# Delta-rule attention and two MLP layers on one core: second half of the sequence written in backward order by the attention itself

## The reference, cut to what matters

```
attention: B, H, S, D = 4, 8, 768, 48
  for t in range(S):                     # state: D x D for each batch and head
      y[t] = q[t] @ state                # the state before key t
      state += beta[t] * outer(k_n[t], v[t] - k_n[t] @ state)
x = y as (B, S, H*D)                     # H*D = 384
layer 1: u = x + (x^T U V)^T;  x = u + relu(u @ w1) @ w2
layer 2: u = x + real(fft2(x)); un = layernorm(u); out = u + relu(un @ w1') @ w2'
```

## Time and profile before

| | us |
|---|---|
| median of 3 runs | 1141.85 |
| lowest and highest | 1141.83, 1143.81 |
| the profiled execution | 1141.97 |
| its span (first to last instruction) | 1140.2 |
| PE busy in the span | 1078.5 (95%) |
| DVE busy | 553.1 (49%) |
| ACT busy | 400.1 (35%) |
| POOL busy | 167.3 (15%) |

### The profile page before, as it was taken

One profiled execution on the slowest core, in us unless ns is written; L12 is line 12 of the kernel. 1 busy time (PEld: TensorE's weight loads), 2 busy tenths in 40 slices (PEclk: granted clock), 3 DMA queues, 4 the chain that ended last, 5 costly groups with the idle time before them and its releaser, 6 DMA issues.

```text
span 1140.2 us, 23939 instructions
## 1 busy us (share of the span) xinstructions
PE 1078.5 (95%) x10258; PEld 1025.4 (90%) x10258; DVE 553.1 (49%) x1094; ACT 400.1 (35%) x759; POOL 167.3 (15%) x213
## 2 busy tenths in 40 slices
PE   2699999999999858999999999999999999999998
PEld 1589889888988848999999999999999999999998
DVE  5677777777777315342232234265334434424222
ACT  1566767666666313231111112123212211211211
POOL 1244444444443200000000000000000000000000
PEclk9999999999999767999999999999999999999999
DMA  5112111122222143311002000022010010000001
GB/s 118 34 30 49 43 45 39 40 47 49 48 50 80 64 115 98 125 42 42 1 1 70 1 1 1 1 67 73 1 43 21 1 35 8 22 21 22 21 22 42
DMA packets 86544, 46.50 MB, mean 41 GB/s; under 512 B 53492, under 2 KB 84776, under 8 KB 86440
## 3 DMA queue, kind: packets, MB, share of 16 engines
q1 hardware_dynamic: 86440, 44.98, 14.1%
HBM read 35.53 MB, written 11.85 MB: 42 GB/s over the span
## 4 chain that ended last, share of the span: by engine, by line
PE 62%; DVE 1%; DMA 1%; SPq 0%; ACT 0%; issue 0%; DVEq 0%
PE dn L1376 9%; PE up L1378 9%; PE up L1376 9%; PE dn L1378 9%; PE up L1377 9%; PE dn L1377 9%; PE sd L1376 2%; PE sd L1377 2%; PE sd L1378 2%; PE sd L1433 1%; PE sd L1420 1%; PE sd L1426 0%; DMA stage<-moe_w_ch 0%; DMA stage<-moe_V 0%; DVE work L1292 0%; PE sd L1445 0%
## 5 line engine op out<-in xcount | busy, mean ns | idle before, releaser
L1280 DVE SCALAR_TENSOR_TENSOR hid_l<-up,hid_h 128x384 fp32r<-128x384 f32 x192 | 107.1, 558 | 378.6 <-ACT hid_h L1227 378.5
L1227 ACT ACTIVATE hid_h<-up 128x384 fp32r<-128x384 f32 x192 | 94.3, 491 | 505.3 <-PE up L1378 505.3
L1376 PE MATMUL dn<-w2h,hid_h 128*128 128x384 f32 x576 | 198.7, 345 | 0.4
L1376 PE MATMUL up<-act_h,w1h 128*128 128x384 f32 x576 | 194.6, 338 | 1.2 <-DVE act_l L1296 1.2
L1378 PE MATMUL up<-act_h,w1l 128*128 128x384 f32 x576 | 195.2, 339 | 0.0
L1377 PE MATMUL up<-act_l,w1h 128*128 128x384 f32 x576 | 194.4, 338 | 0.0
L1377 PE MATMUL dn<-w2l,hid_h 128*128 128x384 f32 x576 | 193.9, 337 | 0.0
L1378 PE MATMUL dn<-w2h,hid_l 128*128 128x384 f32 x576 | 193.7, 336 | 0.0
L1376 PEld LDWEIGHTS up<-act_h,w1h 128*128 128x128 f32 x576 | 109.0, 189 | 2.0 <-DVE act_l L1296 1.6
L388 DVE CAST_PREDICATED zi<-merge_mask,zb 128x512 f16<-128x512 uint8 x144 | 98.9, 695 | 24.5 <-PE zb L662 23.2
L1376 PEld LDWEIGHTS dn<-w2h,hid_h 128*128 128x128 f32 x576 | 108.2, 188 | 2.2 <-issue 1.6
(11 more groups left out here) (142 smaller groups left out, 1595.4 us busy)
## 6 DMA issues: line engine op xcount, KB each, us to landing
stage<-moe_w_ch SPq DMA_DIRECT2D x24, 384.0 KB, 3.8
kq_t<-q_t SPq DMA_DIRECT2D x24, 256.0 KB, 3.4
k_raw<-k SPq DMA_DIRECT2D x24, 192.0 KB, 3.6
v_in<-v SPq DMA_DIRECT2D x24, 192.0 KB, 3.2
x_rows<-x_sb SPq DMA_DIRECT2D x6, 384.0 KB
work<-x_sb SPq DMA_DIRECT2D x4, 576.0 KB, 3.9
work<-x_mem SPq DMA_DIRECT2D x4, 576.0 KB, 5.1
y_mem<-x_sb SPq DMA_DIRECT2D x12, 192.0 KB, 6.9
```

Of the source, the lines that this page charges most:

```text
L1227: nc.scalar.activation(hid_h[:, f % 2], up_b[f % 2][:, 0:HALF], ACT.Relu).then_inc(s_hh, 1)
L1280: nc.vector.scalar_tensor_tensor(hid_l[:, f % 2], up_b[f % 2][:, 0:HALF], 0.0, hid_h[:, f % 2], ALU.max, ALU.subtract).then_inc(s_hl, 1)
L1376: nc.tensor.matmul(bank, ah, bh, start=start, stop=False)
```

## The change

The queries of the second half come in another order: tile c = 3, 4, 5 holds sequence rows 128 * (c + 1) - i for i = 0 to 127, so it runs backward, includes row 128 * (c + 1) and leaves out row 128 * c. The mask of keys against queries for these tiles is `j < C - i`. The output of chunk c goes to tile `tile_of(c)` of `x_sb`: 3, 4, 5 become 5, 4, 3, which is the mirrored order that the layers want. Row 768 does not exist (its queries are zeros); its place in tile 3 is that of row 384. That one row is made apart, from the state before chunk 3: in `update` of steps 6 and 7 PE multiplies one column of queries (`q_mid`) with the state, into row 0 of `cb[g]`, ACT copies it to `x_sb`, and PE waits for this copy before the update. The last chunk's outputs (steps 10 and 11) are added to tile 3, on DVE, which POOL has set to zero at the start.

`mirror_x`, `x_rows`, `x_mem`, `load_x`, `next_x` and POOL's copies are gone. Block 2 reads and updates x in `x_sb`.

```diff
-    gram_mask = np.concatenate([-strict, strict], 1)
+    backward = (j < C - i).astype(np.float32)
+    gram_mask = np.stack([np.concatenate([-strict, m], 1) for m in (strict, backward)], 1)
...
+            sp.dma_start(q_row[:].rearrange("p b a -> p (b a)"), q_mid).then_inc(s_q_row, 16)
             mirror_u(sp, mem)
...
-            for n in range(NC - 1):
-                for g in range(2):
-                    sp.wait_ge(s_y[g], NC + n + 1)
-                mirror_x(sp, mem, x_sb, n)
...
+            last_tile = tile_of(NC - 1) * B * DM
+            nc.gpsimd.memset(x_sb[:, last_tile:last_tile + B * DM], 0.0).then_inc(s_blank, 1)
...
+                def output(g):
+                    if not chain or it < NC - 1:
+                        return
+                    if s == NPAIR - 2:
+                        dve.wait_ge(s_mid_out[g], 2)
+                    x = x_part_of(x_sb, it, 2 * par + g)
+                    nc.vector.tensor_tensor(x, product(5, g), x, ALU.add).then_inc(s_y[g], 1)
...
                 def new_state(g):
                     if not chain:
                         return
+                    output(g)
                     dve.wait_ge(s_c[g], 6 * s + 6)
...
                 def output(g):
...
-                    nc.scalar.copy(x_sb[:, at:at + DM].rearrange("p (h d) -> p h d", h=H), product(5, g)).then_inc(s_y[g], 1)
+                    if it == NC - 1:
+                        return
+                    nc.scalar.copy(x_part_of(x_sb, it, 2 * par + g), product(5, g)).then_inc(s_y[g], 1)
+                    if it == NC // 2:
+                        act.wait_ge(s_blank, 1)
+                        act.wait_ge(s_mid[g], s - NPAIR // 2 + 1)
+                        nc.scalar.copy(x_part_of(x_sb, NC - 1, 2 * par + g)[0:1],
+                                       cb[g][0:1].rearrange("p (h d) -> p h d", h=H)[:, :, 0:D]).then_inc(s_mid_out[g], 1)
...
                     pe.wait_ge(s_y[g], s + 1)
                     pe.wait_ge(s_kb, s + 1)
+                    if it == NC // 2:
...
+                        for p in range(HP):
+                            last = nc.tensor.matmul(
+                                cb[g][0:1, C * p:C * p + C].rearrange("p (o d) -> p o d", d=DP)[:, :, 0:D],
+                                q_row[:, 2 * par + g, p:p + 1], state[:, 2 * par + g, p], start=True, stop=True)
+                        last.then_inc(s_mid[g], 1)
+                        pe.wait_ge(s_mid_out[g], s - NPAIR // 2 + 1)
...
-            sp.wait_ge(s_spill, 16 * (U_MOVES + sum(X_MOVES[:-1])))
-            load_x(0)
+            sp.wait_ge(s_spill, 32)
...
-            mirror_x(sp, side, x_sb, len(X_MOVES) - 1)
...
-            for n in range(B):
-                pool.wait_ge(s_sfree, USE["h", n, ST - 1] + 1)
-                nc.gpsimd.tensor_copy(x_tiles(n), x_now[:]).then_inc(s_keep, 1)
...
-                    nc.vector.tensor_tensor(x_now[:, item[2]], bank_of(item)[:, 0:DM], x_now[:, item[2]],
-                                            ALU.add).then_inc(s_sfree, 1)
+                    xt = x_at(n, item[2])
+                    nc.vector.tensor_tensor(xt, bank_of(item)[:, 0:DM], xt, ALU.add).then_inc(s_sfree, 1)
...
-                if n < B and half == 0:
-                    dve.wait_ge(s_keep, n + 1)
```

More of the change, by code:

```diff
@@ L56, in attn_constants @@
     return {
-        "c_gram": gram_mask,
+        "c_gram": gram_mask.reshape(C, -1),
         "c_merge": merge.reshape(C, -1).view(np.int32),
@@ L76, in by_columns, with tile_of, query_order @@
     return rows.rearrange("s (h c) -> h s c", h=n)
-U_MOVES = 2
-X_MOVES = [3 if c == 0 else 2 for c in range(NC // 2) for par in range(2)]
+def tile_of(c):
+    return c if c < NC // 2 else NC + NC // 2 - 1 - c
+def query_order():
+    forward = np.arange(HALF).reshape(-1, C)
+    backward = C * np.arange(NC // 2 + 1, NC + 1)[:, None] - np.arange(C)[None, :]
+    return np.concatenate([forward, backward]).reshape(-1)
 def mirror_u(sp, mem):
@@ L88, in mirror_u, with attention @@
     sp.dma_start(by_columns(u_mem[1:half], 2), by_columns(u[S - 1:half:-1], 2)).then_inc(mem["s_spill"], 16)
[L91 to L109, removed]
+def attention(nc, ctx, x_sb, q_t, q_mid, k, v, beta, cst, mem):
     def sb(name, shape, dt):
@@ L123, in attention @@
     ident_h = sb("ident_h", [C, C], F16)
-    gram_mask = sb("gram_mask", [C, 2 * C], F32)
+    gram_mask = sb("gram_mask", [C, 2, 2 * C], F32)
+    q_row = sb("q_row", [C, B, HP], F32)
     merge_mask = sb("merge_mask", [C, LEVELS, H * C // 2], U8)
@@ L162, in attention @@
     s_q = [sem(f"s_q{n}") for n in range(NQ)]
+    s_q_row = sem("s_q_row")
     s_v = two("s_v")
@@ L195, in attention @@
     s_y = two("s_y")
+    s_mid = two("s_mid")
+    s_mid_out = two("s_mid_out")
+    s_blank = sem("s_blank")
     s_state = two("s_state")
@@ L246, in _ @@
             sp.dma_start(first_mask[:].rearrange("p a n -> p (a n)"), cst["c_first"].bitcast(U8)).then_inc(s_const, 16)
-            sp.dma_start(gram_mask[:], cst["c_gram"]).then_inc(s_const, 16)
+            sp.dma_start(gram_mask[:].rearrange("p a n -> p (a n)"), cst["c_gram"]).then_inc(s_const, 16)
             sp.dma_start(merge_mask[:].rearrange("p a n -> p (a n)"), cst["c_merge"].bitcast(U8)).then_inc(s_const, 16)
@@ L439, in gram @@
                             nr[:, pp % NQ, g, h], pb[n][:, 256 * u:256 * u + 256],
-                            beta_now[:, par, g, h:h + 1], gram_mask[:], ALU.mult, ALU.mult)
+                            beta_now[:, par, g, h:h + 1], gram_mask[:, int(pp // 2 >= NC // 2)], ALU.mult, ALU.mult)
                     last.then_inc(s_ge, 1)
@@ L976, in mlps @@
     work = sb("work", [C, ST, DM], F32)
-    x_now, rows_n = work, work
+    rows_n = work
     fold = work[:].rearrange("p (a t) d -> p a t d", a=2)
@@ L1431, in side_work @@
                         pe.wait_ge(s_sfree, USE["h", n, ST - 1] + 1)
+                    cols = slice(C * item[3], C * item[3] + C)
                     for t in range(HT):
-                        last = nc.tensor.transpose(bank[:, C * t:C * t + C],
-                                                   work[:, tile(n, item[2], t), C * item[3]:C * item[3] + C], ident[:])
+                        at = tile(n, item[2], t)
+                        rows = rows_n[:, at, cols] if n >= B else x_at(n, at)[:, cols]
+                        last = nc.tensor.transpose(bank[:, C * t:C * t + C], rows, ident[:])
                 elif kind == "A":
@@ L1463, in mlps, with build @@
     pctx.close()
-def build(nc, q_t, k, v, beta, moe_U, moe_V, moe_w_ch1, moe_w_ch2, moe2_w_ch1, moe2_w_ch2,
+def build(nc, q_t, q_mid, k, v, beta, moe_U, moe_V, moe_w_ch1, moe_w_ch2, moe2_w_ch1, moe2_w_ch2,
           c_gram, c_merge, c_first, c_ident, c_dft_s, c_dft_d, out):
@@ L1470, in build @@
         x_sb = ctx.enter_context(nc.sbuf_tensor("x_sb", [C, NC * B * DM], F32))
-        x_rows, x_mem, u_mem, y_mem = [
+        u_mem, y_mem = [
             nc.dram_tensor(name, shape, F32, kind="Internal").ap()
-            for name, shape in (("x_rows", (HALF, B * DM)), ("x_mem", (HALF, B * DM)),
-                                ("u_mem", (HALF, RANK)), ("y_mem", (B, HALF, DM)))]
-        mem = {"U": moe_U, "x_rows": x_rows, "x_mem": x_mem, "u_mem": u_mem,
+            for name, shape in (("u_mem", (HALF, RANK)), ("y_mem", (B, HALF, DM)))]
+        mem = {"U": moe_U, "u_mem": u_mem,
                "s_spill": ctx.enter_context(nc.semaphore("s_spill"))}
         with ExitStack() as own:
-            attention(nc, own, x_sb, q_t, k, v, beta,
+            attention(nc, own, x_sb, q_t, q_mid, k, v, beta,
                       {"c_gram": c_gram, "c_merge": c_merge, "c_first": c_first, "c_ident": c_ident}, mem)
@@ L1495 @@
     arrays = {name: np.ascontiguousarray(inputs[name]) for name in INPUTS}
-    q = arrays.pop("q").reshape(B, HP, 2, NC, C, D).transpose(0, 3, 2, 5, 1, 4)
-    arrays["q_t"] = np.pad(q, ((0, 0),) * 3 + ((0, DP - D),) + ((0, 0),) * 2).reshape(B, NC, C, HP, C)
+    q = np.pad(arrays.pop("q"), ((0, 0), (0, 0), (0, 1), (0, DP - D))).reshape(B, HP, 2, S + 1, DP)
+    arrays["q_t"] = np.ascontiguousarray(q[:, :, :, query_order()].reshape(B, HP, 2, NC, C, DP).transpose(0, 3, 2, 5, 1, 4)
+                                         ).reshape(B, NC, C, HP, C)
+    arrays["q_mid"] = np.ascontiguousarray(q[:, :, :, HALF].transpose(2, 3, 0, 1)).reshape(C, B * HP)
     arrays.update(attn_constants())
```

28 lines of the change are left out of this document (6 added, 22 removed).

## The result

| | before | after |
|---|---|---|
| median, us | 1141.88 (6 runs) | 1151.04 (6 runs) |
| lowest and highest | 1141.12, 1143.81 | 1147.91, 1155.07 |
| the profiled execution | 1141.97 | 1155.07 |
| its span | 1140.2 | 1152.3 |

The ratio is 1.0083, with a 95% interval of 1.0062 to 1.0104: the change makes the kernel slower by 0.8%. The six runs spread over 7.2 us, those of before over 2.7. The profiled execution is the slowest of the six, so its parts add up to more than the median says; I come back to that.

A forecast was written before the change was run, and what follows sets the result against it. PE was taken to set the attention's pace and bound the MLP, with a half-clock serial chain at the attention's end. 1141.97 + 9.9 (terms without the clock) + 6.6 (clock) = 1158.5 us; range 1148 to 1173.

The forecast's parts named there:

- the first rival: The clock holds at full in steps 6 and 7: 1151.9 us, 1148 to 1155 with the bounds; chance 0.34.
- Steps 6 and 7: Attention: ACT waits in order for the single row's products, delaying everything behind; +4.6 us each, +9.2 in all.
- Steps 10 and 11: Attention's end: the output on DVE queues behind the state of g = 1; +0.9 and +1.5 us.
- Start: PE's first work waits for the last constant, behind 128 KB more of mask; +0.5 us, bounds 0 and 1.
- Between the blocks: Without loads of x, SP reaches U 1.4 us sooner and V lands 0.8 sooner (bounds 0 and 1.4); -2.2 us.
- The clock: One fall to half clock in steps 6 and 7, lasting 16 us at factor 1.7; +6.6 us; forecast's chance 0.36.
- The MLP: From 436.4 us on PE is busy 699 of 704 us, so relieving SP, POOL or DMA queues gains nothing.
- The rival on the other side, faster: The two hand-overs per step cost nothing: +0.7 us, at best 1139.4 us in all; chance 0.04.

The follow-up runs named there:

- after_again: The changed kernel run once more, nothing altered; 1151.86 us, ratio 1.0089 to the kernel before.
- The early row: Changed kernel with row 384 multiplied early in steps 6 and 7 into the keys' bank, only the keys' transposes waiting for its copy; 1144.85 us.
- old_loads_ahead: Changed kernel with two 576 KB loads, sized like the old loads of x, put back on SP ahead of U; 1154.35 us (1 run).
- row_triple: Changed kernel with each of the row's four products made three times in the same place; 1157.08 us, ratio 1.0132 to the kernel before.
- best: Changed kernel with row 384 made early, the last outputs on ACT and the backward mask loaded late; 1142.25 us, ratio 0.9991 to the kernel before.
- best_dve: As best, but DVE, not ACT, puts row 384 in its place in steps 10 and 11; 1142.15 us, ratio 1.0000 to the kernel before.
- best_fill: As best_dve, with PE's products for row 384 put where PE waits for 0.2 us anyway; 1139.78 us, ratio 0.9986 to the kernel before.
- last_on_act: Changed kernel with the outputs of steps 10 and 11 back on ACT, row 384 waiting in a small buffer, POOL's memset gone; 1149.17 us.

## Why the prediction was right or wrong

The direction and the range held: 1151.04 in 1148 to 1173. The forecast of 1158.5 was 7.5 us too high, and the time is that of the first rival, 1151.9. That the rival comes so close is partly luck: the gap between the blocks gave back 1.7 us more than its term, and against that stood what the rival had left out, the clock: 1.2 us at the start of after_again, and 1.5 to 2.6 us for each fall in steps 6 and 7 of other executions. The bounds "1148 to 1155" beside it are not the sum of the terms' bounds either, which runs from 1147.2 to 1157.1. Against the profile without falls in steps 6 and 7 (after_again, span 1148.89, 8.7 us over before), by the terms of the sum:

- **Steps 6 and 7, +9.2 predicted:** 4.58 and 4.57, so +9.15. The mechanism was right in each link: ACT waits in its order, `halve(1)` and `n_turned(1)` are late, PE gets the delay twice. PE's piece was 0.82 for my 0.85. ACT's copy of one partition took 0.47, against 0.46 to 0.50 for 128 partitions with as many elements in each. With 0.10 us an instruction PE's piece lies between the two rows, as I had taken it. By the Trainium skill ("TensorE: Matmul & The Clock Gate", LDWEIGHTS and Back-to-back issue gap) I had estimated 0.34 for the piece, with the gap given there for a single matmul by itself; the trace doesn't agree. The early row shows that the place was two thirds of the cost, and the work one third.
- **Steps 10 and 11, +2.4 predicted:** +2.4 (60.27 for 57.91), of which the order of the output is 2.0 to 2.1; the rest goes with 0.8 us more of half clock (24.4 for 23.6).
- **Start, +0.5 predicted:** not shown. The first output copy of after_again came 1.2 us later than before's although PE's first work began on time, at 7.64: that was the clock. In the profile of after PE began at 8.43, 0.8 late. Over all profiles the means with the mask in front and with half of it late differ by 0.5, within their scatter.
- **Between the blocks, -2.2 predicted:** -3.9, the term most mis-sized without the clock. The issue of the two loads was right with 1.4. V's landing was -1.4 and not -0.8: it fell to the lower bound. And the 0.8 us by which SP's two issues of U became shorter were no term at all. I had taken the durations of SP's issues from the row as if they were its own; old_loads_ahead shows that they were longer because of the two loads in front of them. The last 0.3 is about what the second weight chunk landed sooner (3.23 us for 3.56).
- **The clock, +6.6 predicted:** the step that failed. The falls do happen, in the steps that I named, and at the point that I named or up to 1 us behind it, but not in every execution: in three of the seven profiles that keep the row in its place they are in both steps, in one (row_triple) in one step, in three in none. And a fall costs 1.5 to 2.6 us, as the clock came back after 3.4 or 6.8 us, not after 16. What failed is the length: "about half of such a step" had no row behind it. The factor of 1.7 was near: it gives 1.4 and 2.8 us for 3.4 and 6.8 us of half clock, and the profile of after has 1.5 and 2.4. How much of the median the falls are is not known. The median of after_again is 1151.86 and its profiled execution, without a fall in the two steps, 1150.68, 1.2 us less; but that one had lost 1.2 us by the clock at its start. The Trainium skill's account of a clock sent down and up by short, frequent idle moments ("TensorE: Matmul & The Clock Gate", A second HAM failure mode) is borne out in four of the seven profiles: in the timeline of PE in step 6 above no wait is over 0.65 us, and the clock fell and came back. In the other three the same kind of waits left it at full.
- **The MLP, 0 predicted:** 703.65 for 703.78 us. What left POOL, SP and the DMA engines there was worth nothing.

The rival on the other side, faster, needed hand-overs that cost nothing. They cost 3.1 us a step. But with the row out altogether (no_row) the kernel is at 0.9987 of before, some 1.5 us faster, where I had +0.7 for free hand-overs (no_row leaves out the row's work as well): what the change gains elsewhere is real, and small.

## What to carry to other kernels

When a small extra result is fetched between two engines, ask what stands behind the wait on the engine that copies: a wait of an in-order engine for a later instruction of another hands the delay to everything behind it, and here that was 3.1 of 4.6 us a step. Make such a result early, into a bank that is free then, and let only the next user of the bank wait. A transfer taken away in front of a serial chain gives back more than its issue: here what was behind it landed sooner, and the two issues right behind it got shorter.

## What I had not expected of the hardware

SP's time to issue a DMA can depend on what it issued before. The same load of U took 1.03 us behind the two loads of x, 1.04 in old_loads_ahead, and 0.38 with nothing ahead. Only two issues were longer: the third, of the identity, took 0.49 for 0.48 us, and V's four took 1.82 us in both cases, although the second load of 576 KB was still under way then (it took 5.3 us to land). So a queue that is merely busy does not explain it; the mechanism is open.

An instruction fetch may lie on the path. In best the DMA list of the stretch in which V lands has one, and in best_dve as well (queue and kind: packets, MB, share of the 16 engines' time, from 415 to 420 us):

```profile
q1 hardware_dynamic: 1301, 0.89, 68.1%
q8 instruction: 1, 0.02, 1.8%
```

The second line is a single packet of 16 KB, which kept one of the 16 DMA engines for 1.47 us (1.12 in best_dve). V's last part landed after 4.15 and 3.69 us there, and the gap was 23.1 and 22.55. In the eight other profiles without it in that stretch (best_fill apart) and without loads of x ahead, V took 2.12 to 2.25. In last_on_act the fetch came 0.5 us later and V landed as usual, after 2.13, but the first weight chunk after 5.1 us for 3.3. In best_fill, which differs from best_dve only in the order of PE's work, the fetch is not in this stretch and V took 2.12 (chain that ended last; start and duration):

```profile
418.29 2.12 DMA stage<-moe_V
423.47 3.07 DMA stage<-moe_w_ch
```

All three profiles with a fetch among these loads have a late landing, two of V and one of the weight chunk; that the fetch is the cause was not tested by itself, nor which engine's code it is.
